# Finding the largest |w| of two weight matrices beside attention: half of the pieces on VectorE, one piece every three units, and the maximum shared through free columns of another bank

## The chip, the core and the metric

The kernel runs on one core of a Trainium2 chip. The metric is the device time of one execution in microseconds. Three runs of the kernel before gave 901.03 us (median), 900.47 and 902.3 us. The profile is of one further execution, which took 900.44 us; its span, from the first to the last recorded instruction, is 898.5 us, so 1.94 us lie outside the span.

The engines are called TensorE (PE in the rows, with PEld for its weight loads), ScalarE (ACT), VectorE (DVE), GpSimd (POOL) and SyncE (SP), which issues most transfers.

## What is computed

```python
def reference(q, k, v, n_global, n_local, x.. w_in, w_out, domain_probs, w1, w2):
    # 1. attention, 2 batches x 8 heads, 768 positions, 64 wide, a mask of a band and some global keys
    scores = q @ k.T / 8 + bias(slope of the head, distance);  a = softmax(where(keep, scores, -1e9))
    x = (a @ v) as 1536 x 512
    # 2. feed-forward, w_in 512 x 2048, w_out 2048 x 512
    h = x @ w_in;  x = (h * tanh(softplus(h))) @ w_out
    # 3. four experts, w1 512 x 1024, w2 1024 x 512 each, weighted by normalised domain_probs
    out = sum_e p[:, e] * (relu(x @ w1[e]) @ w2[e])
```

All inputs are 32-bit. The kernel computes a product of 32-bit matrices as three products of 16-bit parts: each operand is scaled by a power of two, its value rounded to 16 bits is the high part, and what is left is the low part. The scale needs the largest absolute value of the matrix, which is what the change is about.

## The kernel before, in words

**Attention.** There are 8 pairs of heads (`PAIRS`), numbered 0 to 7, and each pair has 12 units (`UNITS`): one unit is one head's block of 128 queries. A unit's number in the whole stage is 12 x pair + u, from 0 to 95. For each unit TensorE makes the scores (line 548), VectorE adds the bias and takes the row maximum (`biased`, L1122), ScalarE takes the exponential (`expo`, L858), TensorE transposes the result (`turn`, L586), ScalarE writes the high part of the transpose (L897), VectorE the low part (L1234), and TensorE multiplies with the values (`pv`, L605). ScalarE and VectorE work two units ahead with the exponentials; three buffers of scores and two banks of transposes (banks 4 and 5, one for even and one for odd units) hold the pipeline. All engines take their instructions in the written order. In units 0, 2, 4 and 6 of a pair TensorE also transposes pieces of the next pair's q and k into bank 3 (`fill`, L503), which ScalarE copies out (L848, L851). At the end of each half pair VectorE divides by the row sums (`output`, L1154, L1158, L1162). From pair 4 on, TensorE also turns a quarter of the first attention rows for the next stage (`turn_x`, L511), in units 56, 68, 80 and 87, with a high part from ScalarE (L932) and a low part from VectorE (L1219).

**The two weight matrices.** `w_in` lies in `stage`, `w_out` in `wB`, each as 8 pieces (`PIECES`) of 128 x 1024. ScalarE takes |w| of one piece with a running sum (`weights_sum`, L872; the sum bounds the maximum) in each of units 21 to 28 for `w_in` and 33 to 40 for `w_out`: a table of first units, `W_SUMS`. VectorE takes the largest of the 8 results (`weights_max`, L1082). In unit 32 or 44 (`W_SHARE`) TensorE multiplies this column with the identity into bank 3, so that each partition has all 128 values; in unit 34 or 46 (`W_SCALE`) VectorE takes their maximum (L1174) and makes the scale in a chain of four dependent operations on one column (`make_scale`, L1062 to L1065). The first fill of pairs 4 and 5 waits for that, since it writes bank 3 again.

**The splits.** GpSimd waits for the scale (`w_scale`) and then splits the 8 pieces of `w_in`, and after them the 8 of `w_out`, each in three operations: scale (L781), high part (L784), low part (L787). TensorE needs the parts of `w_in` (`w_split` at 1) from unit 93, and those of `w_out` (`w_split` at 2) before the first `second_product`.

**Feed-forward.** A step T has 12 matmuls of `first_product` (L615) and, from T = 6, 12 of `second_product` (L687) of the step T - 6. Between them an activation chain runs in order: ScalarE exponential (L975), VectorE `min` (L1351) and product (L1353), ScalarE logarithm and exponential (L991, L993), VectorE two products (L1365, L1367), GpSimd a product (L824), ScalarE high part (L985), VectorE low part (L1359). VectorE also takes the product with the bank (L1372). After T = 1 and T = 3 TensorE turns the second and third group of attention rows (16 transposes each, L511); their low parts (four times L1219) stand on VectorE after the L1372 of the same step. The second `turn_x` waits for the low parts of the first, and `second_product(0)` for those of the second.

## Time and profile before

| | value |
|---|---|
| device time, median of 3 runs | 901.03 us (900.47 to 902.3) |
| profiled execution | 900.44 us, span 898.5 us |
| TensorE matmul busy in the span | 872.5 us, 97% |
| VectorE, ScalarE, GpSimd busy | 482.7, 319.0, 260.9 us |
| chain that ended last, by engine | PE 89%, ACT 5%, DVE 3% |

The attention stage ends at about 148 us of the span and the feed-forward stage's start at about 167 us; from there TensorE is never idle for long. The slices of the page show where TensorE is less than full: the first one (start), slices 2 to 7, and the start of the feed-forward. To place a unit in the trace, take the fourth fill of a pair (`fill`, k = 3, two transposes), which stands in u = 6: unit 18 is at 39.92 us, unit 30 at 59.57, unit 42 at 80.11, unit 54 at 94.65 and unit 66 at 109.01 us.

### The profile page before, as it was taken

What the parts mean: (1) busy time and instruction counts of PE and PEld (TensorE: products, weight loads), DVE (VectorE), ACT (ScalarE), POOL (GpSimd) and SP (SyncE); (2) the same over time, 40 slices, a digit from 0 to 9 for tenths busy, and PEclk for the clock granted to TensorE, in tenths of its full rate; (3) what the DMA queues carried; (4) which work ended last, traced back from release to release, by engine and by line L of the source; (5) the groups of instructions that cost most, each with busy time, mean ns of one, the idle gap of its engine ahead of it and who ended that gap; (6) DMA issues with size and microseconds to landing.
All of it is one profiled execution on the core that took longest, in us unless ns stands there. A gap on an engine that the chain in (4) does not pass through costs nothing.

```text
span 898.5 us, 12643 instructions
## 1 busy us (share of the span) xinstructions
PE 872.5 (97%) x4918; PEld 444.0 (49%) x4918; DVE 482.7 (54%) x1008; ACT 319.0 (35%) x596; POOL 260.9 (29%) x222
## 2 busy tenths in 40 slices
PE   6988999999999999999999999999999999999998
PEld 5766876444444444444444444444444444444443
DVE  7756887999999989874442125222134321212121
ACT  4898886545554655542021010102010111101020
POOL 1659992222222222210039200077000292000000
PEclk8988999999999999999999999999999999999999
DMA  9961510000000000202100500001300000000001
GB/s 213 307 209 37 168 59 1 1 1 1 1 7 4 0 1 1 97 1 94 10 1 0 187 1 1 6 0 63 124 1 7 0 0 0 0 24 23 35 12 49
DMA packets 52004, 39.19 MB, mean 44 GB/s; under 512 B 40816, under 2 KB 41712, under 8 KB 51440
## 3 DMA queue, kind: packets, MB, share of 16 engines
q1 hardware_dynamic: 49888, 34.31, 12.9%
q10 hardware_dynamic: 2064, 4.19, 1.3%
q8 instruction: 31, 0.51, 0.2%
q14 instruction: 21, 0.17, 0.1%
HBM read 35.35 MB, written 3.15 MB: 43 GB/s over the span
## 4 chain that ended last, share of the span: by engine, by line
PE 89%; ACT 5%; DVE 3%; issue 1%; SPq 1%; DMA 0%; POOL 0%; DVEq 0%
PE bank L615 68%; PE bank L687 14%; PE bank L548 2%; PE bank L586 2%; ACT scaled L872 2%; PE bank L605 2%; ACT tmp L858 1%; ACT tmp L897 1%; PE bank L503 1%; DVE xT L1219 1%; SPq L420 1%; DMA xT<-in_v 0%; DVE tmp L1122 0%; ACT hid L848 0%; DVE tmp L1234 0%
## 5 line engine op out<-in xcount | busy, mean ns | idle before, releaser
L966 ACT ACTIVATE hid<-bank 128x512 f16<-128x512 f32 x96 | 57.3, 597 | 422.2 <-PE bank L615 422.2
L615 PE MATMUL bank<-xT,wA 128*128 128x512 f16 (+1 forms) x864 | 194.7, 379 | 0.0
L1344 DVE SCALAR_TENSOR_TENSOR hid<-bank,hid 128x512 f16<-128x512 f32 x96 | 66.4, 692 | 181.7 <-ACT hid L966 181.7
L615 PEld LDWEIGHTS bank<-xT,wA 128*128 128x128 f16 x864 | 84.4, 98 | 100.6
L687 PE MATMUL bank<-hid,wB 128*128 128x512 f16 x576 | 132.2, 379 | 0.9 <-DVE xT L1219 0.9
L615 PE MATMUL bank<-xT,wB 128*128 x576 | 125.3, 379 | 0.0
L615 PE MATMUL bank<-wB,hid 128*128 128x512 f16 x576 | 125.3, 379 | 0.0
L615 PE MATMUL bank<-wA,hid 128*128 128x512 f16 x576 | 125.3, 379 | 0.0
L824 POOL TENSOR_TENSOR tmp<-tmp 128x512 f32<-128x512 f32 x48 | 61.5, 1281 | 189.9 <-DVE tmp L1367 189.9
L781 POOL TENSOR_SCALAR stage<-stage,sc 128x1024 f32<-128x1024 f32 x32 | 36.0, 1125 | 260.4 <-DVEq L1337 250.4
L1424 DVE SCALAR_TENSOR_TENSOR acc<-bank,pg,acc 128x512 f32<-128x512 f32 x36 | 27.0, 750 | 131.7 <-PE bank L615 131.7
L687 PEld LDWEIGHTS bank<-hid,wB 128*128 128x128 f16 x576 | 56.3, 98 | 69.1 <-DVE xT L1219 1.4
L615 PEld LDWEIGHTS bank<-wA,hid 128*128 128x128 f16 x576 | 56.4, 98 | 67.9
L615 PEld LDWEIGHTS bank<-wB,hid 128*128 128x128 f16 x576 | 56.4, 98 | 68.0
L615 PEld LDWEIGHTS bank<-xT,wB 128*128 128x128 f16 x576 | 56.3, 98 | 68.0
L1234 DVE SCALAR_TENSOR_TENSOR tmp<-bank,tmp 128x384 f16<-128x384 f32 (+2 forms) x96 | 47.0, 490 | 32.8 <-ACT tmp L897 31.4
L615 PE MATMUL bank<-xT,hid 128*128 (+1 forms) x288 | 63.6, 379 | 0.0
L586 PE MATMUL bank<-ident,tmp 128*128 128x128 f32 x240 | 46.8, 296 | 8.0 <-DVE tmp L1234 5.0
L985 ACT ACTIVATE hid<-tmp 128x512 f16<-128x512 f32 x48 | 30.2, 629 | 68.0 <-POOL tmp L824 67.9
L858 ACT ACTIVATE tmp<-tmp 128x288 f32<-128x288 f32 (+2 forms) x96 | 48.5, 506 | 13.8 <-DVE tmp L1122 12.6
L615 PEld LDWEIGHTS bank<-xT,hid 128*128 128x128 f16 x288 | 28.2, 98 | 34.0
L975 ACT ACTIVATE tmp<-bank,sc 128x512 f32<-128x512 f32 x48 | 32.6, 682 | 33.4 <-PE bank L615 30.3
(113 smaller groups left out, 949.1 us busy)
## 6 DMA issues: line engine op xcount, KB each, us to landing
stage<-in_moe_w SPq DMA_DIRECT2D x8, 2048.0 KB, 9.8
stage<-in_moe_w_in SPq DMA_DIRECT2D x1, 4096.0 KB, 14.5
wB<-in_moe_w_out ACTq DMA_DIRECT2D x1, 4096.0 KB, 16.4
hid<-in_q SPq DMA_DIRECT2D x16, 192.0 KB, 3.4
hid<-in_k SPq DMA_DIRECT2D x16, 192.0 KB, 3.6
xT<-in_v SPq DMA_DIRECT2D x8, 384.0 KB, 5.1
out_y<-acc SPq DMA_DIRECT2D x12, 256.0 KB, 2.0
rows<-max SPq DMA_DIRECT2D x4, 128.0 KB, 4.3
```

Of the source, the lines that this page charges most:

```text
L586: last = pe.transpose(dst[:, b * P:(b + 1) * P], src[:, b * P:(b + 1) * P], ident[:])
L615: last = pe.matmul(dst, lhs(c, a), rhs(c, b), start=(c == 0 and n == 0), stop=(c == chunks - 1 and n == 2))
L687: last = pe.matmul(psum(4 + d), w_out_s[:, a, f // 2, f % 2, d * P:(d + 1) * P], hv[:, T % RING, b, :], start=(f == 0 and n == 0), stop=(f ...
L781: pool.tensor_scalar(tmp, src, scale, 1.0, ALU.mult, ALU.mult).then_inc(w_part, 1)
L824: pool.tensor_tensor(g_t[T % 4], g_t[T % 4], r_t[T % 2], ALU.mult).then_inc(g_ready, 1)
L858: act.activation(t, t, ACT.Exp, bias=nmax[:, u:u + 1], scale=-1.0).then_inc(p_ready, 1)
L966: act.activation(hv[:, f, 0, :], psum(f % 4), ACT.Relu).then_inc(f_hi, 1)
L975: act.activation(u_t[T % 2], psum(T % 4), ACT.Exp, scale=inv_h).then_inc(u_ready, 1)
L985: act.activation(hv[:, m % RING, 0, :], g_t[m % 4], ACT.Copy).then_inc(h_hi, 1)
L1234: dve.scalar_tensor_tensor(pt[:, 1], src, P_SCALE, pt[:, 0], ALU.mult, ALU.subtract).then_inc(pT_dve, 1)
L1344: dve.scalar_tensor_tensor(hv[:, f, 1, :], psum(f % 4), 0.0, hv[:, f, 0, :], ALU.max, ALU.subtract).then_inc(f_ready, 1)
L1424: last = dve.scalar_tensor_tensor(y, psum(4 + j), pg[:, j:j + 1], y, ALU.mult, ALU.add)
```

## The change

For each matrix the first four pieces of |w| stay on ScalarE, and the last four go to VectorE as a reduction with the largest absolute value (new function `weights_part_max`). They no longer stand in consecutive units: ScalarE takes `w_in` in units 22, 28, 34, 40 and `w_out` in 46, 52, 58, 64 (`W_ACT`), VectorE three units after each, in 25, 31, 37, 43 and 49, 55, 61, 67 (`W_DVE`). The maximum of the pieces is taken in unit 44 or 68, and shared and turned into a scale in unit 47 or 71, where TensorE writes it into columns 384 to 511 of the unit's own transpose bank, directly ahead of the transposes. The waits on bank 3 go away. (The branch for a mask that is not banded is changed too; these inputs don't take it.)

```diff
-        W_SUMS = ({0: 21, 1: 33}, {0: UNITS})
-        W_MAX = ({n: at + PIECES for n, at in W_SUMS[0].items()}, {0: UNITS + PIECES})
-        W_SHARE = ({0: 2 * UNITS + 8, 1: 3 * UNITS + 8}, {0: UNITS + 9})
-        W_SCALE = ({n: at + 2 for n, at in W_SHARE[0].items()}, {0: UNITS + 10})
+        BY_ACT, BY_DVE = range(PIECES // 2), range(PIECES // 2, PIECES)
+        W_ACT = [[2 * n * UNITS + 2 * UNITS - 2 + 6 * c for c in range(PIECES // 2)] for n in range(2)]
+        W_DVE = [[at + 3 for at in units] for units in W_ACT]
+        W_MAX = ({n: units[-1] + 1 for n, units in enumerate(W_DVE)}, {0: UNITS + 8})
+        W_SHARE = ({n: at + 3 for n, at in W_MAX[0].items()}, {0: UNITS + 9})
...
                 if banded and k == 0 and isinstance(m, int):
-                    if m in (4, 5):
-                        pe.wait_ge(w_scale, m - 3)
                     if m >= PAIRS - 2:
...
+                if banded:
+                    for n, unit in W_SHARE[0].items():
+                        if at == unit:
+                            share_max(n, psum(4 + u % 2, P, 3 * P))
                 for b in range(len((band if banded else full)[u // 2])):
                     last = pe.transpose(dst[:, b * P:(b + 1) * P], src[:, b * P:(b + 1) * P], ident[:])
...
+            def weights_part_max(n, c):
+
+                if c == BY_DVE[0]:
+                    dve.wait_ge(w_out_loaded if n else w_loaded, 16)
+                    if n:
+                        dve.wait_ge(w_max, n)
+                src = w_out_raw if n else stage
+                dve.tensor_reduce(wpieces[:, c:c + 1], src[:, c * PIECE:(c + 1) * PIECE], AX_X, ALU.max,
+                                  apply_absolute_value=True).then_inc(w_part_max, 1)
...
+            def matrix_max(n, src):
+
                 dve.wait_ge(max_psum, n + 1)
-                link(dve.tensor_reduce(scale_cols(col)[0], psum(3, P), AX_X, ALU.max))
-                make_scale(link, scale_cols(col), 10)
+                first = 2 * SCALE_STEPS + 1 + (SCALE_STEPS + 1) * n
+                chain(scale_step, first)(dve.tensor_reduce(scale_cols((SC_WIN, SC_WOUT)[n])[0], src, AX_X, ALU.max))
+
+            def matrix_scale(n):
+
+                link = chain(scale_step, 2 * SCALE_STEPS + 2 + (SCALE_STEPS + 1) * n)
+                make_scale(link, scale_cols((SC_WIN, SC_WOUT)[n]), 10)
                 dve.sem_inc(w_scale, 1)
```

ScalarE around units 21 to 24. Before, each exponential (L858) is followed by a piece (L872):

```order
65 L897 ACTIVATE tmp<-bank2 128x384 [waits pT_psum]
66 L858 ACTIVATE tmp<-tmp 128x288 [waits s_ready]
67 L872 ACTIVATE scaled,wpieces<-stage 128x1024 [waits w_sum,w_loaded]
68 L897 ACTIVATE tmp<-bank2 128x384 [waits pT_psum]
69 L858 ACTIVATE tmp<-tmp 128x128 [waits s_ready]
70 L872 ACTIVATE scaled,wpieces<-stage 128x1024 [waits w_sum]
71 L897 ACTIVATE tmp<-bank2 128x384 [waits pT_psum]
72 L858 ACTIVATE tmp<-tmp 128x128 [waits s_ready]
73 L872 ACTIVATE scaled,wpieces<-stage 128x1024 [waits w_sum]
```

After, in the same place of the program (L905 is what was L897, L864 what was L858, L880 the piece):

```order
65 L905 ACTIVATE tmp<-bank2 128x384 [waits pT_psum]
66 L864 ACTIVATE tmp<-tmp 128x288 [waits s_ready]
67 L905 ACTIVATE tmp<-bank2 128x384 [waits pT_psum]
68 L864 ACTIVATE tmp<-tmp 128x128 [waits s_ready]
69 L880 ACTIVATE scaled,wpieces<-stage 128x1024 [waits w_sum,w_loaded]
70 L905 ACTIVATE tmp<-bank2 128x384 [waits pT_psum]
71 L864 ACTIVATE tmp<-tmp 128x128 [waits s_ready]
72 L905 ACTIVATE tmp<-bank2 128x128 [waits pT_psum]
73 L864 ACTIVATE tmp<-tmp 128x256 [waits s_ready]
```

One piece stands where three stood; the next follows six units later.

VectorE at the end of pair 3. Before, the scale of `w_out` is made in unit 46 (row 208 is that unit's low part):

```order
208 L1234 SCALAR_TENSOR_TENSOR tmp<-bank2,tmp 128x384 [waits pT_act]
209 L1174 TENSOR_REDUCE sc<-bank1 128x1 [waits max_psum]
210 L1062 TENSOR_SCALAR sc<-sc 128x1 [waits scale_step]
211 L1063 TENSOR_SCALAR sc<-sc 128x1 [waits scale_step]
212 L1064 TENSOR_SCALAR sc<-sc 128x1 [waits scale_step]
213 L1065 TENSOR_SCALAR sc<-sc 128x1 [waits scale_step]
214 L1162 TENSOR_TENSOR acc<-bank3,tmp 128x384 [waits scale_step,o_step]
```

After, what stands there is the scale of `w_in`, in unit 47, around that unit's low part (L1265):

```order
207 L1179 TENSOR_TENSOR acc<-bank3,tmp 128x384 [waits o_step]
208 L1139 ISA tmp<-bank0,tmp 128x128 [waits s_psum]
209 L1139 ISA tmp 128x1
210 L1191 TENSOR_REDUCE sc<-bank2 128x1 [waits max_psum,pT_act]
211 L1265 SCALAR_TENSOR_TENSOR tmp<-bank2,tmp 128x384 [waits scale_step]
212 L1068 TENSOR_SCALAR sc<-sc 128x1
213 L1069 TENSOR_SCALAR sc<-sc 128x1 [waits scale_step]
214 L1070 TENSOR_SCALAR sc<-sc 128x1 [waits scale_step]
215 L1071 TENSOR_SCALAR sc<-sc 128x1 [waits scale_step]
```

The scale of `w_in` has moved from unit 34 to unit 47, and that of `w_out` from unit 46 to unit 71. GpSimd's own list of instructions is the same in both kernels; its first split waits for the scale of `w_in`.

## Rows read from the trace of the kernel before

**Rows 1.** Windows, one per pair: start:end, us, busy (x count) by engine, granted clock, DMA.

```profile
39.92:59.57 19.65, 16.35 (x176) 13.27 (x173) 11.01 (x42) 19.11 (x45) 15.82 (x23) 0.83 0.85 264
59.57:80.11 20.54, 16.68 (x175) 13.59 (x175) 11.96 (x49) 19.33 (x45) 12.51 (x9) 0.83 0.17 39
80.11:94.65 14.54, 13.61 (x174) 11.30 (x174) 12.11 (x49) 11.85 (x29) 14.03 (x11) 1.00 0.25 57
94.65:109.01 14.36, 13.78 (x179) 11.48 (x176) 11.71 (x43) 12.27 (x30) 13.66 (x11) 1.00 0.60 175
```

**Rows 2.** Timeline, attention: start, us, engine, line, operation, tiles [idle before <-releaser].

```profile
44.24 1.04 ACT L872 ACTIVATE scaled<-stage 128x1024 f32<-128x1024 f32 x1
...
45.18 0.19 ACT L872 ACTIVATION_READ_ACCUMULATOR scaled<-stage 128x1 f32 x1
...
92.60 0.53 ACT L858 ACTIVATE tmp<-tmp 128x288 f32<-128x288 f32 x1
...
93.94 0.52 PE L586 MATMUL bank<-ident,tmp 128*128 128x128 f32 x3
...
101.82 0.40 ACT L858 ACTIVATE tmp<-tmp 128x128 f32<-128x128 f32 x1 [1.22 <-DVE tmp L1122]
```

**Rows 3.** Timeline of VectorE: the chain, unit 47's low part, and a reduction.

```profile
85.49 0.28 DVE L1174 TENSOR_REDUCE sc<-bank 128x1 f32<-128x128 f32 x1
...
87.34 0.55 DVE L1234 SCALAR_TENSOR_TENSOR tmp<-bank,tmp 128x384 f16<-128x384 f32 x1
...
180.13 1.21 DVE L1072 TENSOR_REDUCE wpieces<-stage 128x1 f32<-128x1024 f32 x1
```

**Rows 4.** Timeline of GpSimd: first split of each matrix, first feed-forward product.

```profile
67.09 1.12 POOL L781 TENSOR_SCALAR stage<-stage,sc 128x1024 f32<-128x1024 f32 x1 [9.97 <-DVEq L1176]
...
102.71 1.13 POOL L781 TENSOR_SCALAR scaled<-wB,sc 128x1024 f32<-128x1024 f32 x1
...
153.51 1.27 POOL L824 TENSOR_TENSOR tmp<-tmp 128x512 f32<-128x512 f32 x1 [14.31 <-DVE tmp L1367]
```

**Rows 5.** Timeline at the start of the feed-forward, VectorE and TensorE.

```profile
149.16 0.43 DVE L1351 TENSOR_SCALAR tmp<-tmp 128x512 f32<-128x512 f32 x1 [0.82 <-ACT tmp L975]
...
149.95 5.34 PE L615 MATMUL bank<-xT,wA 128*128 128x512 f16 x24
...
152.74 0.69 DVE L1367 SCALAR_TENSOR_TENSOR tmp<-xT,tmp 128x512 f32<-128x512 f32 x1
...
153.95 2.47 DVE L1219 TENSOR_TENSOR xT<-bank,xT 128x512 f16<-128x512 f32 x4
...
156.57 1.94 PE L511 MATMUL bank<-ident,acc 128*128 128x128 f32 x16 [1.28 <-DVE xT L1219]
...
158.34 7.93 PE L615 MATMUL bank<-xT,wA 128*128 128x512 f16 x36
...
167.20 2.76 PE L687 MATMUL bank<-hid,wB 128*128 128x512 f16 x12 [0.93 <-DVE xT L1219]
```

**Rows 6.** Timeline, later stretches: VectorE and GpSimd at the same time.

```profile
174.95 1.27 POOL L824 TENSOR_TENSOR tmp<-tmp 128x512 f32<-128x512 f32 x1 [3.47 <-DVE tmp L1367]
...
175.39 1.11 DVE L1351 TENSOR_SCALAR tmp<-tmp 128x512 f32<-128x512 f32 x1
...
301.88 1.27 POOL L824 TENSOR_TENSOR tmp<-tmp 128x512 f32<-128x512 f32 x1 [3.46 <-DVE tmp L1367]
...
302.31 1.38 DVE L1294 SCALAR_TENSOR_TENSOR xT<-acc,sc,xT 128x512 f16<-128x512 f32 x1
...
605.69 1.12 POOL L781 TENSOR_SCALAR stage<-stage,sc 128x1024 f32<-128x1024 f32 x1
...
605.91 0.93 DVE L1401 TENSOR_SCALAR pg<-pr,sc 128x4 f32<-128x4 f32 x1
```

**Rows 7.** Windows of 4 us, same columns: TensorE's clock after a wait.

```profile
50.00:54.00 4.00, 2.58 (x14) 2.02 (x13) 1.60 (x8) 4.00 (x10) 3.67 (x6) 0.62 1.08 385
54.00:58.00 4.00, 4.00 (x31) 3.36 (x27) 2.19 (x7) 4.00 (x10) 2.89 (x5) 0.53 0.53 130
```

More of the change, by code:

```diff
@@ L550, in scores_of_two, with share_max @@
                             last.then_inc(s_psum, 1)
-            def share_max(n):
+            def share_max(n, dst=psum(3, P)):
                 pe.wait_ge(w_max, n + 1)
-                pe.matmul(psum(3, P), wpart[:, 0:1].to_broadcast([P, P]), ident[:], start=True, stop=True
+                pe.matmul(dst, wpart[:, 0:1].to_broadcast([P, P]), ident[:], start=True, stop=True
                           ).then_inc(max_psum, 1)
@@ L907, in pair @@
                         load_w_out()
-                    for n, start in W_SUMS[0 if banded else 1].items():
-                        if at - start in range(PIECES):
-                            if n and at == start:
-                                act.wait_ge(w_max, n)
-                            weights_sum(n, at - start)
+                    for n in range(2 if banded else 1):
+                        units = W_ACT[n] if banded else W_FULL
+                        if at in units:
+                            weights_sum(n, units.index(at))
                     if at + 1 in V_SUMS:
@@ L921, in pair @@
                     load_w_out()
-                    act.wait_ge(w_max, 1)
-                    for c in range(PIECES):
+                    for c in BY_ACT:
                         weights_sum(1, c)
@@ L1168, in first @@
                     biased(0, 0, 1, banded)
[L1170 to L1172 removed]
+            def matrix_max(n, src):
                 dve.wait_ge(max_psum, n + 1)
[L1174 to L1175 removed]
+                first = 2 * SCALE_STEPS + 1 + (SCALE_STEPS + 1) * n
[3 more added lines that the diff above has]
+                make_scale(link, scale_cols((SC_WIN, SC_WOUT)[n]), 10)
                 dve.sem_inc(w_scale, 1)
             def matrix_step(m, u, banded):
[L1181 to L1186 removed]
+                at = m * UNITS + u
+                for n in range(2 if banded else 1):
+                    units = W_DVE[n] if banded else W_FULL
+                    if at in units:
+                        weights_part_max(n, BY_DVE[units.index(at)])
+                    if at == W_MAX[0 if banded else 1][n]:
+                        weights_max(n)
+                    if banded and at == W_SHARE[0][n]:
+                        matrix_scale(n)
+                if not banded and at == W_SCALE_FULL:
+                    matrix_max(0, psum(3, P))
+                    matrix_scale(0)
             def values_low():
@@ L1232, in pair @@
                     dve.wait_ge(pT_act, base + u + 1)
+                    if banded:
+                        for n, unit in W_SHARE[0].items():
+                            if (2 * i + slot) * UNITS + u == unit:
+                                matrix_max(n, psum(4 + u % 2, P, 3 * P))
                     src, pt = p_out(u, banded)
@@ L1444, in _ @@
                 dve.sem_inc(tables_free, 1)
+                for c in BY_DVE:
+                    weights_part_max(1, c)
                 weights_max(1)
-                matrix_scale(1, SC_WOUT)
+                matrix_max(1, psum(3, P))
+                matrix_scale(1)
                 rest()
```

19 lines of the change are left out of this document (9 added, 10 removed).

## The prediction

> **What bounds the kernel now.** I read the slices first: TensorE is full from 167 us to the end, so a gain must come from the stages ahead of that, and what counts is when TensorE starts `second_product(0)`, at 167.20 us [rows 5]. Everything behind it follows one for one. Next I cut attention into windows, one per pair, from fourth fill to fourth fill [rows 1]. The two windows that hold the 16 pieces take 19.65 and 20.54 us, and ScalarE is busy for 19.11 and 19.33 us of them: it is the bound there, each piece being 1.04 + 0.19 us of its time [rows 2]. The windows without pieces take 14.54 and 14.36 us with TensorE busy for 13.6 and 13.8: TensorE is the bound, with ScalarE at 11.9 to 12.3 and VectorE at 11.7 to 12.1 us. Third, the timeline from 148 to 167 us [rows 5]: VectorE goes from L1351 at 149.16 to L1367 at 152.74, then L1372 and four L1219 that end at 156.42, and only then may TensorE turn x again, having waited since 155.29 (149.95 + 5.34). VectorE is the bound of this stretch. Fourth, GpSimd's timeline [rows 4]: it starts to split at 67.09, takes 35.62 us for `w_in` (to 102.71), and is done at 139.20 (153.51 less an idle time of 14.31), 72.1 us after its start and 10 us ahead of that VectorE chain.
>
> **What attention gains.** A pair without pieces, scale or x costs about 13.6 us: the window from 94.65 (14.36) less 0.44 us of `turn_x` on TensorE and a third of a microsecond for L1219; TensorE's busy time of 13.61 in the third window is the floor. From unit 18 (39.92) to unit 54 (94.65) there are 54.73 us; three such pairs are 40.8, so 13.9 us are extra. Two scale chains are in it, at 14.54 - 13.6 = 0.9 us each; the 16 pieces cost 12.1 us, 0.75 us each.
>
> After the change a piece stands alone. On ScalarE it takes 1.23 us, on VectorE 1.21 us, by the same kind of reduction [rows 3]. What of it reaches TensorE depends on the lead: an exponential ends at 93.13 and its transpose starts at 93.94 [rows 2], a lead of 0.8 us, so 0.4 to 0.5 us of a lone piece come through. Four of ScalarE's pieces (u = 10) fall close to the pair's end, where it waits 1.22 us for VectorE anyway [rows 2]; against that, VectorE's pieces in u = 1 come when it is late already. Bounds: 0.2 us each if only busy time counts (11.85 + 2 x 1.23 = 14.3 against 13.6 is 0.7 us for a pair's four pieces), 0.75 us as today. I take 0.45, nearest to the lead's row. The scale chains now stand after unit 47's and unit 71's low part, at the pair's end where VectorE is late, and one of them behind an L1219: 1.1 us each. Extra time after: 16 x 0.45 + 2 x 1.1 = 9.4 us. **Attention ends 13.9 - 9.4 = 4.5 us earlier.** The shared matmul (0.24 us of TensorE's time) stays; the waits of two fills on bank 3 go, and the fills stood at pair ends which VectorE holds back all the same, so I give nothing for them.
>
> **What it costs: GpSimd starts late.** The split waits for the scale of `w_in`, now in unit 47. Before, unit 42's fill is at 80.11 and unit 47's low part at 87.34 [rows 3], 7.2 us later with a chain of 0.9 ahead of it, so 6.3 without. After: 39.92 + 2 x 13.6 + 9 pieces x 0.45 + 6.3 = 77.5; the maximum (0.28), the low part (0.55) and the chain with its signal (1.1; before, all this but the low part went from 85.49 to about 86.6) give 79.4. GpSimd starts 12.3 us later than at 67.09 and is done, if undisturbed, at 139.2 + 12.3 = 151.5. The scale of `w_out` (unit 71, some 112 us) is in time for 79.4 + 35.6 = 115.0. TensorE's use of the `w_in` parts from unit 93 on (136 us or later) is covered too, and `w_out`'s parts are needed only at 167. The transfers of the first expert's weights, which SyncE issues behind `w_split`, move to 115 us and have 50 us of room.
>
> But VectorE's chain L1351 to L1367 now begins at 149.16 - 4.5 = 144.7, while GpSimd is still splitting, 6.8 us long. In the trace the two collide [rows 6]: L1351 beside a GpSimd product takes 1.11 us and not 0.43; L1294, with two inputs in SBUF, takes 1.38 and ends 0.54 us after GpSimd's operation ends; a TENSOR_SCALAR of only four elements takes 0.93 us and ends 0.03 us after GpSimd's L781. So VectorE operations of these two kinds wait until the GpSimd operation is over. The Trainium skill (SBUF — State Buffer, "SBUF: two separate sides") calls this an exclusive lock on a shared port pair, taken by whoever starts first and held for the whole instruction; all three pairs of rows agree with it.
>
> L1351, L1353, L1351, L1353, L1365, L1367 are all of these kinds; L1372 and L1219 read one input from PSUM and are not. I lay them out against GpSimd's operations of 1.12, 1.05 and 2.13 us, taking turns. GpSimd's last four operations start, undisturbed, at 144.8 (2.13), 147.1, 148.3 and 149.4 (2.13). VectorE: L1351 waits to 144.8, ends 145.2; GpSimd to 147.3; L1353 to 148.0; GpSimd to 149.1, with L1372 under it; L1351 to 149.5; GpSimd to 150.6; L1353 to 151.3; GpSimd to 153.4, its last; L1365 to 154.0, L1367 to 154.7. Before, L1367 ended at 153.4. **The 4.5 us are gone, and VectorE is 1.3 us later than before.** In general, a piece cheaper by 0.1 brings attention forward by 1.6 us but GpSimd's end by only 0.9 us, and it is GpSimd's end that now sets this point: L1367's end is 150.65 + 9 x (cost of a piece), 152.5 for 0.2 and 157.4 for 0.75.
>
> **And TensorE cools down.** The four L1219 now end at 156.4 + 1.3 = 157.7, but TensorE has done its 24 matmuls at 155.3 - 4.5 = 150.8: it idles for 6.9 us where it idled for 1.28. Attention shows what follows a thin stretch: in 50 to 54 us, with TensorE 65% busy after the waits for ScalarE, the granted clock is 0.62, and in 54 to 58 us, with TensorE busy throughout, 0.53 [rows 7], near the lower of its two levels (1.2 against 2.4 GHz). Read as a share of time at half clock, the two rows make 3.0 + 3.8 = 6.8 us, some 5.5 of them work. I take 5.5 us of work at half speed, 2.75 us lost; the bounds are nothing and all 6.8 us, 3.4 lost. TensorE then needs 1.77 us for the 16 transposes (156.57 to 158.34), 7.93 for 36 matmuls and the 2.75, and is at `second_product(0)` at 157.7 + 0.15 + 12.45 = 170.3. Before it was 167.2, of which 0.93 was a wait for VectorE, so the loss of the clock is hidden for that much. The result is **+3.1 us**: 903.5 for a profiled execution like the one at 900.44, 904.1 on the median of 901.03.
>
> **The rivals.**
> (a) The collision costs little: the splits' operations leave VectorE its turn, or VectorE's reads pass beside them. Against it stand all of [rows 6]. Then only GpSimd's first product is late: ready at 149.0, started at 151.5, 2.5 us, of which 1.3 are slack (ScalarE's exponential of T = 1 ended at 156.7, VectorE used it at 158.0). Gain 4.5 - 1.2 = 3.3 us: 897.7. Chance 0.14. The skill's lock is what speaks against this one.
> (b) Collision as forecast, but TensorE keeps its clock or regains it at once: VectorE's 1.3 us is all, 902.3. For it: 97% busy around. Against: a wait of 6.9 us is longer than any inside attention. Chance 0.18.
> (c) The pieces are nearly hidden (0.2 us each or less): GpSimd starts 2.3 us earlier, result 3.1 - 9 x 0.25 = +0.8, 901.9. For it: the pieces' positions. Chance 0.13.
> (d) The pieces cost as much as today, 0.7, because VectorE has no lead to spare either: attention gains 0.5, and the result is 3.1 + 9 x 0.25 = +5.4, 906.4. Chance 0.12.
> The forecast itself, between (c) and (d) with the clock lost, has 0.43.
>
> **How the numbers follow.** Predicted 904.1 us. The range must reach from near (a) to (d): 899 to 907 leaves out most of (a) and a little above (d). A measurement of this kernel can tell about 0.2%, 1.8 us, from no change: faster is below 899.2, slower above 902.8. Slower: forecast 0.42, (d) 0.12, part of (b) 0.06, together 0.60. Same: (b) 0.12, (c) 0.12, 0.01 of each of two others, together 0.26. Faster: (a), 0.14.
>
> **What the profile would show.** Windows of the pairs 1 to 5 at 15 to 16 us with the clock at 1.00 throughout (pieces at 0.45); one at 14 speaks for (c), one above 16.5 for (d). GpSimd's first split at 79 to 80 us, its last one ending after 152. L1351, L1353, L1365 and L1367 of the first two steps longer than 0.43 and 0.69 us, each ending shortly after a GpSimd operation; if they keep their times, (a). TensorE's idle time ahead of its second group of L511 near 7 us, and a clock of about 0.5 behind it; if 1.00, (b). The forecast is wrong if L1367's first end is earlier than 153 us, or if the feed-forward later loses or regains time behind 170 us, where I expect none.

## The result, and the profile after

The changed kernel takes 902.46 us (median of 22 executions, 901.21 to 903.93); the kernel before, run beside it, takes 900.69. The ratio is 1.0013, 95% interval 1.0007 to 1.0019: 1.2 us slower by the ratio and 1.8 by the medians, small but clear of the noise, within the 0.2% that the prediction calls no change, and inside the forecast range. The profiled execution took 903.18 us, 2.7 more than the profiled one of before (900.44); the first is the third slowest of its 22 and the second the third fastest of its 22, so this pair shows more than the typical difference.

In these two executions the whole difference lies ahead of `second_product(0)`: TensorE starts it at 169.79 against 167.20, 2.59 us later, and from there to the end of the span both need 731.3 to 731.4 us.

Windows of the changed kernel, one per pair (units 18 to 78, from fourth fill to fourth fill), columns as in [rows 1]:

```profile
40.26:55.30 15.04, 13.61 (x176) 11.10 (x173) 11.97 (x42) 13.35 (x33) 13.80 (x20) 1.00 0.98 324
55.30:70.83 15.53, 13.65 (x172) 11.12 (x173) 13.15 (x45) 13.55 (x33) 2.02 (x4) 1.00 0.30 69
70.83:87.71 16.88, 13.91 (x175) 11.39 (x175) 14.13 (x51) 13.48 (x33) 7.79 (x6) 1.00 0.21 48
87.71:103.67 15.96, 14.27 (x176) 11.67 (x177) 13.66 (x46) 14.04 (x34) 15.36 (x12) 1.00 0.23 52
103.67:121.46 17.79, 15.81 (x178) 13.00 (x178) 13.91 (x52) 12.17 (x30) 17.01 (x13) 0.90 0.27 99
```

The two windows of 19.65 and 20.54 us are gone, and ScalarE is no longer full in any. The five windows come to 81.20 us; before, from 39.92 to unit 78's fill at 123.37, they came to 83.45, so these units take 2.25 us less. Unit 18, ahead of which no piece lies, came 0.34 us later in this execution (40.26), which leaves attention 1.9 us ahead at unit 78, not 4.5. The last window has a granted clock of 0.90. The windows of 4 us show where:

```profile
112.00:116.00 4.00, 2.65 (x27) 2.35 (x28) 2.98 (x17) 2.46 (x6) 3.92 (x3) 0.92 0.00 0
116.00:120.00 4.00, 4.00 (x31) 3.24 (x31) 2.23 (x8) 2.35 (x7) 3.73 (x4) 0.66 0.81 286
```

Then the end of attention, timeline of GpSimd and VectorE together (L1350 is before's L1319; L1382, L1384, L1396, L1398, L1403 are L1351, L1353, L1365, L1367, L1372; L787 to L793 are L781 to L787, the three operations of a split; L1246 is L1219), to be held against [rows 4, 5]:

```profile
79.58 1.12 POOL L787 TENSOR_SCALAR stage<-stage,sc 128x1024 f32<-128x1024 f32 x1 [22.11 <-DVEq L1197]
...
144.97 2.13 POOL L793 TENSOR_TENSOR wB<-scaled,wB 128x1024 f16<-128x1024 f32 x1
147.20 1.12 POOL L787 TENSOR_SCALAR scaled<-wB,sc 128x1024 f32<-128x1024 f32 x1
148.41 1.09 POOL L790 TENSOR_SCALAR wB<-scaled 128x1024 f16<-128x1024 f32 x1
149.59 2.45 POOL L793 TENSOR_TENSOR wB<-scaled,wB 128x1024 f16<-128x1024 f32 x1
```

```profile
146.10 1.02 DVE L1350 TENSOR_TENSOR sc<-sc 128x1 f32<-128x1 f32 x1
147.15 0.16 DVE L1351 TENSOR_TENSOR sc<-sc 128x1 f32<-128x1 f32 x1
148.13 0.48 DVE L1382 TENSOR_SCALAR tmp<-tmp 128x512 f32<-128x512 f32 x1 [0.81 <-ACT tmp L981]
148.64 1.40 DVE L1384 SCALAR_TENSOR_TENSOR tmp<-tmp 128x512 f32<-128x512 f32 x1
150.08 0.69 DVE L1403 SCALAR_TENSOR_TENSOR tmp<-bank,tmp 128x512 f32<-128x512 f32 x1
150.68 1.63 DVE L1382 TENSOR_SCALAR tmp<-tmp 128x512 f32<-128x512 f32 x1
152.35 0.69 DVE L1384 SCALAR_TENSOR_TENSOR tmp<-tmp 128x512 f32<-128x512 f32 x1
152.96 0.69 DVE L1396 SCALAR_TENSOR_TENSOR xT<-tmp 128x512 f32<-128x512 f32 x1
153.68 0.69 DVE L1398 SCALAR_TENSOR_TENSOR tmp<-xT,tmp 128x512 f32<-128x512 f32 x1
```

GpSimd starts 12.5 us later than before and is still at work when attention ends. L1350, one column that takes 0.15 us alone, takes 1.02 and ends at 147.12, 0.02 after GpSimd's product (147.10). It stands ahead of ScalarE's exponential, so of the 1.9 us by which attention is ahead only 1.0 is left when the chain starts (148.13 against 149.16). L1384 takes 1.40 in place of 0.69 and ends 0.54 after GpSimd's L790; L1382 takes 1.63 in place of 0.43 and ends 0.27 after GpSimd's last operation (152.04). Operations behind 152.04 have their old times. L1403, which reads a bank of PSUM, has its 0.69 beside GpSimd. So the chain's last end is 154.37 against 153.43 before.

The timeline of TensorE behind it, and its clock:

```profile
148.04 5.34 PE L621 MATMUL bank<-xT,wA 128*128 128x512 f16 x24
157.51 3.64 PE L513 MATMUL bank<-ident,acc 128*128 128x128 f32 x16 [4.12 <-DVE xT L1246]
160.94 9.02 PE L621 MATMUL bank<-xT,wA 128*128 128x512 f16 x36
```

```profile
152.00:156.00 4.00, 1.38 (x7) 0.41 (x5) 3.93 (x7) 2.24 (x5) 1.30 (x2) 1.00 0.00 0
156.00:160.00 4.00, 2.49 (x12) 2.52 (x13) 3.93 (x8) 2.19 (x4) 0.00 (x0) 0.54 0.02 6
160.00:164.00 4.00, 4.00 (x16) 2.08 (x15) 3.60 (x6) 2.24 (x4) 1.27 (x1) 0.61 0.00 0
```

TensorE waits for 4.12 us where it waited for 1.28, and the granted clock falls to 0.54 and 0.61, near the lower of its two levels. The 16 transposes take 1.70 us longer than before and the 36 matmuls 1.09; the wait of 0.93 that stood ahead of `second_product(0)` is gone. 0.94 + 2.79 - 0.93, less 0.2 by which the groups of matmuls overlap in the rows, is the 2.59.

### The profile page after: what moved, and what is told of

Its sections match the earlier page's. It is cut to its first block, busy times and chain, and to the rows that moved or that the text cites. A ratio compares the mean times of both kernels' runs of the same rounds, so it can differ in the third digit from the quotient of the medians.

```text
span 901.2 us, 12640 instructions
## 1 busy us (share of the span) xinstructions
PE 872.5 (97%) x4918; PEld 443.6 (49%) x4918; DVE 493.3 (55%) x1016; ACT 311.2 (35%) x580; POOL 261.3 (29%) x222
## 4 chain that ended last, share of the span: by engine, by line
PE 88%; DVE 5%; ACT 5%; issue 2%; POOL 0%; DVEq 0%
PE bank L621 68%; PE bank L693 14%; ACT tmp L864 2%; PE bank L550 1%; ACT tmp L905 1%; PE bank L592 1%; PE bank L611 1%; DVE tmp L1139 1%; ACT scaled L880 1%; DVE wpieces L1088 1%; PE bank L505 1%; PE bank L569 1%; DVE tmp L1265 1%; DVE xT L1246 1%; PE bank L513 1%
## 5 line engine op out<-in xcount | busy, mean ns | idle before, releaser
L787 POOL TENSOR_SCALAR stage<-stage,sc 128x1024 f32<-128x1024 f32 x32 | 36.0, 1125 | 272.6 <-DVEq L1368 250.4
L1265 DVE SCALAR_TENSOR_TENSOR tmp<-bank,tmp 128x384 f16<-128x384 f32 (+2 forms) x96 | 47.0, 490 | 21.3 <-ACT tmp L905 19.3
L864 ACT ACTIVATE tmp<-tmp 128x288 f32<-128x288 f32 (+2 forms) x96 | 48.4, 505 | 18.9 <-DVE tmp L1139 18.1
```

The costliest lines, as they stand in the source:

```text
L787: pool.tensor_scalar(tmp, src, scale, 1.0, ALU.mult, ALU.mult).then_inc(w_part, 1)
L864: act.activation(t, t, ACT.Exp, bias=nmax[:, u:u + 1], scale=-1.0).then_inc(p_ready, 1)
L1265: dve.scalar_tensor_tensor(pt[:, 1], src, P_SCALE, pt[:, 0], ALU.mult, ALU.subtract).then_inc(pT_dve, 1)
```

## The experiments

The kernels of experiments 1 to 4, 5 to 8, 9 and 10, and 11 and 12 were each run beside the kernel before on one chip; its medians there were 901.14, 900.62, 900.75 and 900.99, and the ratios below are against it. "Changed" is the changed kernel.

**1. The collision alone: before, with GpSimd made late.**

```diff
             pool.wait_ge(w_scale, 1)
+            pool.wait_ge(pT_dve, 44)
```

> The kernel before, with one more wait: GpSimd, when it has the scale of w_in, also waits until VectorE has written the low part of unit 43 (pT_dve at 44, some 81.5 us). Attention's own work is as before. Theory (collision): the split ends, undisturbed, near 81.6 + 72.1 = 153.7 us, 4.5 us into VectorE's chain that begins at 149.16; L1351 and L1353 of the first steps grow beyond 0.43 and 0.69 us, L1367's first end moves from 153.4 to 156 or later, TensorE waits 4 to 5 us ahead of its second group of transposes and its clock falls; second_product(0) moves from 167.2 to 171 to 172 us, the kernel takes 4 to 5 us more (905). Rival (no collision, only a late start of GpSimd's first product): the split ends where the first product starts anyway, 153.5 us, so the time stays within 1 us of 900.7.

904.82 us, ratio 1.0039 (1.0027 to 1.0051). GpSimd's first split came at 83.55 and its last operation ended at 155.90. Timelines of VectorE and TensorE:

```profile
149.40 1.61 DVE L1320 TENSOR_TENSOR sc<-sc 128x1 f32<-128x1 f32 x1
...
152.51 1.40 DVE L1354 SCALAR_TENSOR_TENSOR tmp<-tmp 128x512 f32<-128x512 f32 x1
```

```profile
161.38 3.19 PE L511 MATMUL bank<-ident,acc 128*128 128x128 f32 x16 [4.70 <-DVE xT L1220]
```

With nothing of the change but a late start (3.9 us later than in the changed kernel, at GpSimd's end), the same operations are long by the same amounts, L1354 by 1.40 and the second L1352 by 1.63, TensorE waits 4.70 us, and its clock falls (0.73 in 160 to 164 us; the transposes take 3.19 us and not 1.94). The ratio makes it 3.5 us. `second_product(0)` came 5.4 us later than before in the profiled execution, 1.4 of which were there at unit 42 already (fill at 81.49 against 80.11), before GpSimd's first split. The collision is a cause of its own.

**2. The collision away: the changed kernel with GpSimd's last two pieces of `w_out` set to zero and not split** (that part of the output's work is left out).

```diff
+                if c < PIECES - 2: split(...)
+                else: pool.memset(hi, 0.0); pool.memset(lo, 0.0)
```

> The kernel after, but GpSimd fills the parts of w_out's last two pieces with zeros (memset) in place of splitting them, so its work ends some 7 to 9 us earlier, near 143 to 145 us, before VectorE's chain begins at 148 us; the feed-forward is computed with a part of w_out missing. Nothing else changes. Theory (collision): L1382 and L1384 (before: L1351, L1353) are back at 0.43 and 0.69 us, L1398's first end moves from 154.4 to 151.5 us, TensorE's wait ahead of its second group of transposes falls from 4.1 to about 1.3 us, the clock stays at 1.00, and second_product(0) starts at 165.3 in place of 169.8: 898.7 us, 2 us faster than before. Rival (the late feed-forward start has another cause, such as TensorE's clock alone): it stays at 169 to 170 and the time at 902 to 903.

898.39 us, ratio 0.9962 (0.9946 to 0.9977). GpSimd is done at 145.98 and VectorE's chain has its old durations:

```profile
146.93 0.43 DVE L1386 TENSOR_SCALAR tmp<-tmp 128x512 f32<-128x512 f32 x1 [0.81 <-ACT tmp L985]
```

```profile
154.33 1.94 PE L513 MATMUL bank<-ident,acc 128*128 128x128 f32 x16 [1.27 <-DVE xT L1250]
```

Without GpSimd beside the chain the change would be a gain of 2.7 us by the medians. The loss hangs on GpSimd's row, and attention's gain is real.

**3. The clock away: 16 spare matmuls for TensorE between its `first_product` and its wait.**

```diff
+                    if T == 3:
+                        pe.wait_ge(b_ready, 1)
+                        for _ in range(16):
+                            pe.matmul(psum(0), w_in_s[:, 0, 0, 0:P], xs(0, 0, 0), start=True, stop=True)
```

> The kernel after with 16 spare matmuls of 512 columns on TensorE behind the first_product of T = 3, in the time in which it waits for VectorE (4.1 us; the 16 take 3.5 us at full clock), into a bank that is free. Results are not touched. Theory (part of the loss is TensorE's clock after that wait): the granted clock stays at 1.00 in 156 to 164 us, the second group of transposes takes 1.8 us and not 3.4, and second_product(0) starts at 168.1, bounded by VectorE, 1.7 us earlier than 169.8; the time falls by 1.7 us against after, to 900.8 to 901.4. Rival (the clock is hidden, VectorE's chain is the bound all the way): second_product(0) stays at 169.8.

901.09 us, ratio 0.9998 (0.9988 to 1.0007). Windows of two pairs, timeline of TensorE, and that of VectorE:

```profile
54.97:70.50 15.53, 13.64 (x173) 11.12 (x173) 13.16 (x45) 13.54 (x33) 2.00 (x4) 1.00 0.31 69
...
103.32:119.54 16.22, 14.26 (x179) 11.82 (x179) 13.84 (x52) 12.27 (x30) 15.53 (x12) 1.00 0.22 68
```

```profile
151.29 3.62 PE L747 MATMUL bank<-xT,wA 128*128 128x512 f16 x16
156.64 1.94 PE L513 MATMUL bank<-ident,acc 128*128 128x128 f32 x16 [1.74 <-DVE xT L1250]
...
167.27 2.77 PE L693 MATMUL bank<-hid,wB 128*128 128x512 f16 x12 [0.92 <-DVE xT L1250]
```

```profile
145.46 1.49 DVE L1386 TENSOR_SCALAR tmp<-tmp 128x512 f32<-128x512 f32 x1 [0.81 <-ACT tmp L985]
146.98 1.49 DVE L1388 SCALAR_TENSOR_TENSOR tmp<-tmp 128x512 f32<-128x512 f32 x1
...
149.11 0.54 DVE L1386 TENSOR_SCALAR tmp<-tmp 128x512 f32<-128x512 f32 x1
149.68 2.50 DVE L1388 SCALAR_TENSOR_TENSOR tmp<-tmp 128x512 f32<-128x512 f32 x1
...
152.81 0.69 DVE L1402 SCALAR_TENSOR_TENSOR tmp<-xT,tmp 128x512 f32<-128x512 f32 x1
```

The clock stayed at 1.00, here and, by itself, at 112 to 120 us as well, where the code is the changed kernel's. So this execution shows both sums clean: attention's five windows take 79.60 us, a gain of 3.85, VectorE's chain starts 3.7 us earlier than before, and it ends at 153.50 against 153.43. In it the first L1386 loses 1.06 us, the first L1388 0.80, the second L1386 0.12 and the second L1388 1.81: 3.8 in all. All that attention gained is eaten by the collision, to 0.1 us.

**4. GpSimd early: the table with pieces every two units at times, `w_in` done at unit 35.**

```diff
+        W_ACT = [[21,25,29,33],[40,46,52,58]]
+        W_DVE = [[23,27,31,35],[43,49,55,61]]
+        W_MAX = ({0: 36, 1: 62}, {0: UNITS + 8})
+        W_SHARE = ({0: 39, 1: 64}, {0: UNITS + 9})
```

> The kernel after with another table: w_in's pieces every two units from 21 (ScalarE 21, 25, 29, 33, VectorE 23, 27, 31, 35), its maximum in 36 and its scale in 39, in the middle of a pair; w_out's pieces every three units from 40 (ScalarE 40, 46, 52, 58, VectorE 43, 49, 55, 61), maximum in 62, scale in 64, also mid-pair. Theory: the pieces cost about 0.5 us each as in after (7.7 to 8.5 us in all), the two chains, which in after cost 1.4 us (unit 47) and 3.0 us (unit 71) at pair ends, cost 0.3 each in the middle where VectorE has time; attention ends 4.5 to 5.5 us earlier than before. GpSimd starts at 65 to 67 us and ends by 139, so nothing collides at 143 us: second_product(0) at 162 to 163 us, the kernel at 896 us (895.5 to 897.5). Rival (chains cost the same anywhere, or pieces every two units cost 0.75 as in before): attention ends 1 to 2.5 us earlier, 898 to 900 us.

900.15 us, ratio 0.9986 (0.9977 to 0.9995): a little better than before, but I had expected far more. GpSimd started at 71.92, ended at 144.83, and nothing collided. But the first two windows took 17.03 and 19.00 us:

```profile
39.63:56.66 17.03, 13.82 (x175) 11.22 (x172) 13.08 (x43) 13.36 (x33) 15.65 (x23) 1.00 0.98 314
56.66:75.66 19.00, 14.24 (x178) 11.54 (x174) 14.10 (x51) 14.56 (x35) 3.71 (x5) 0.99 0.19 42
```

Less the bare pair of 13.6 that is 0.7 us for each of five pieces, and, if the scale chain costs 1.4 here too, 1.0 for each of four; what the chain costs in mid-pair was not measured by itself. A piece two units behind another costs as much as one in a row of ScalarE's did, or more. The third window had its clock down (0.82) and took 17.69. VectorE's last chain began at 150.14, 1 us later than before and not 4 earlier, and that is where the gain from the missing collision went.

**5. The shared maximum of `w_in` back in bank 3.**

```diff
+                    if m == 5:
+                        pe.wait_ge(w_scale, 1)
-                        if at == unit:
+                        if n and at == unit:
```

> The kernel after with one part undone: the maximum of w_in (not of w_out) is shared through bank 3 again, by a matmul behind unit 45, and the first fill of the next pair (unit 48) waits for the scale; VectorE still takes its maximum and makes the scale in unit 47. Theory (the chain's cost is VectorE's time at the pair's end, the bank matters little): the pair from unit 42 to 54 takes 16.9 us as in after, plus at most 0.4 us for the fill that waits; the time is that of after within 0.5 us. Rival (the waits on bank 3 were a part of what the change gains): the pair takes 1 us more or longer, the kernel 903.5 or more.

901.80 us, ratio 1.0017 (1.0006 to 1.0028), the changed kernel's within 0.7. The window from unit 42's fill was 1.2 us longer in the profiled execution, as the rival had it, but with a granted clock of 0.72 at 78 to 84 us. So what the free columns are worth by themselves is not settled; by the times it is small.

**6. What VectorE's pieces cost: the changed kernel without its eight reductions** (their maxima are set to 0).

```diff
-                dve.tensor_reduce(wpieces[:, c:c + 1], src[...], AX_X, ALU.max, ...)
+                dve.memset(wpieces[:, c:c + 1], 0.0)
```

> The kernel after with VectorE's eight pieces left out (zeros in their place, so the scales rest on half of each matrix); ScalarE's eight stay where they are. One look at attention. Theory (a lone piece costs about 0.47 us on either engine): the pairs from unit 18, 30, 42 and 54 take 0.5 to 1 us less each than in after (15.4, 15.5, 16.9, 16.0): near 14.7, 14.6, 15.9, 15.0. Rival (ScalarE's pieces are hidden by its waits at pair ends, VectorE's cost it all): 13.8, 13.7, 15.1, 14.5. Rival (VectorE's are hidden): as in after.

One execution, 900.20 us, which the time alone can't be judged by. Windows of two pairs:

```profile
54.61:69.18 14.57, 13.44 (x173) 11.02 (x173) 11.20 (x45) 13.44 (x33) 2.41 (x4) 1.00 0.34 78
69.18:85.16 15.98, 13.68 (x175) 11.29 (x175) 12.16 (x51) 13.44 (x33) 7.38 (x6) 1.00 0.23 52
```

Two reductions fewer make the first 0.96 us shorter than in experiment 3: 0.48 us each. Between these two windows lies a scale chain, 15.98 - 14.57 = 1.4 us. VectorE's last chain now begins at 142.52, 6.6 us earlier than before, and ends at 151.43 beside GpSimd (done at 150.16): only 2.0 us of 6.6 are left. GpSimd's end sets this point, as the prediction's sum has it.

**7. The scale of `w_in` three units earlier.**

```diff
+        W_ACT = [[21,27,33,39],[45,51,56,61]]
+        W_DVE = [[24,30,36,42],[48,53,58,63]]
+        W_MAX = ({0: 42, 1: 63}, {0: UNITS + 8})
+        W_SHARE = ({0: 44, 1: 65}, {0: UNITS + 9})
```

> The kernel after with another table: pieces still one every three units, but from unit 21 on (w_in: ScalarE 21, 27, 33, 39, VectorE 24, 30, 36, 42), its scale in unit 44 and not 47; w_out's from 45 (ScalarE 45, 51, 56, 61, VectorE 48, 53, 58, 63), its scale in unit 65, in the middle of a pair, and not in 71. Theory (GpSimd's end sets the start of the feed-forward, and chains at a pair's end cost 1.4 us and a fall of the clock): GpSimd starts near 75.5, not 79.3, and ends near 148 us; pieces cost 0.47 each as in after, the chains 0.3 to 0.9, so VectorE's chain begins near 144 us (5 us earlier than before), collides for 4 us, and L1398's first end is near 150.5 to 151 us, 2.5 us earlier than before; the clock does not fall at 112 us. If the clock also holds in the wait of some 3.5 us ahead of the second transposes, 898.2 us; if it falls there, 899.9. Rival (attention's end alone counts): 895.7 us. Rival (GpSimd's end does not matter, as VectorE waits for something else): no better than after, 902.

903.55 us, ratio 1.0030 (1.0018 to 1.0041), a clear miss. GpSimd ended at 150.65, ahead of the chain, but attention lost more than that gave:

```profile
55.82:72.95 17.13, 14.03 (x173) 11.27 (x173) 12.89 (x44) 13.32 (x33) 0.80 (x3) 1.00 0.21 47
```

This window holds four pieces, three units apart, as does the one of 15.53. From 55.5 to 72.9 us ScalarE waits 3.5 us for VectorE's L1139, in six units, against 1.7 us in three in the changed kernel. Where a piece stands within the pair matters as much as how many there are. `second_product(0)` began at 169.81, as late as in the changed kernel, here without a collision.

**8. The same with 12 spare matmuls** (the edit of experiment 3, 12 for 16).

> e6_scale_44 with 12 spare matmuls of 512 columns (2.6 us) on TensorE behind the first_product of T = 3. Theory (clock): the granted clock is 1.00 from there on in every execution, so the slower ones of e6 go: 898.2 us and a narrower spread. Rival (the clock holds by itself, or the spare work delays the transposes): equal to e6 or slower by up to 1 us.

904.06 us, ratio 1.0031 (1.0019 to 1.0044). Nothing to win: in experiment 7's profiled execution the clock at the start of the feed-forward was 1.00 already. Of the two kernels that got spare matmuls, they paid in the one whose clock had fallen there.

**9. Parity or place: the changed table moved two units earlier.**

```diff
+        W_ACT = [[20,26,32,38],[44,50,56,62]]
+        W_DVE = [[23,29,35,41],[47,53,59,65]]
+        W_MAX = ({0: 42, 1: 66}, {0: UNITS + 8})
+        W_SHARE = ({0: 45, 1: 69}, {0: UNITS + 9})
```

> The changed kernel with its whole table of pieces moved two units earlier: ScalarE's at units 20, 26, 32, 38 and 44, 50, 56, 62, VectorE's at 23, 29, 35, 41 and 47, 53, 59, 65, the two chains at 45 and 69. Spacing and the split between the engines stay as they are; ScalarE's pieces stay at even units and VectorE's at odd ones, but they stand at other places of the head pair (ScalarE 8 and 2, VectorE 11 and 5 in place of 10 and 4, 1 and 7). It asks why the run with pieces at 21, 27, 33, 39 had a second window of 17.13 us against 15.53. Theory A, that it is the parity (which engine's piece falls on the even units): this table costs what the changed kernel's costs, the window from unit 30's fill to unit 42's stays near 15.5, GpSimd starts its splits two units (2.6 us) earlier, near 77.0, and ends near 149.4, so that about half of the collision with VectorE's chain goes; 901.4, 1.0 under the changed kernel in the same call. Theory B, that it is the place in the pair: windows near 17, GpSimd from 78.5 on, and 903.5.

902.93 us, ratio 1.0022 (1.0014 to 1.0031). The second window is 16.34 us, GpSimd starts at 79.05, only 0.5 earlier than in the changed kernel though its signal stands two units earlier. The parity is as in the changed kernel and the window is 0.8 us longer, so the place counts, as theory B has it; but 16.34 lies halfway between 15.53 and 17.13, so the place alone is shown for half of that difference. Here TensorE itself waits longer (2.2 us for L1139 and 2.1 for L1265 between 40 and 72 us, against 0.6 each in the changed kernel); which unit's neighbours make a place cheap I have not found out.

**10. Two of GpSimd's pieces held back.** Pieces 6 and 7 of `w_out` are read only from `second_product(12)` on.

```diff
+            HELD = {4: PIECES - 2, 8: PIECES - 1}
+            for c in range(PIECES - len(HELD)):
+                w_out_piece(c)
             pool.sem_inc(w_split, 1)
             for T in range(STEPS):
                 pool.wait_ge(q_ready, T + 1)
                 pool.tensor_tensor(g_t[T % 4], g_t[T % 4], r_t[T % 2], ALU.mult).then_inc(g_ready, 1)
+                if T in HELD:
+                    w_out_piece(HELD[T])
...
+                    if g == 0 and f in (FT - 4, FT - 2):
+                        pe.wait_ge(w_out_part, f // 2 + 1)
```

> The changed kernel with GpSimd's last two pieces of w_out not split before the first feed-forward products but behind GpSimd's products of steps 4 and 8, while the matmuls of the second product that read them wait for them at steps 12 and 14. Nothing is left out. GpSimd's row of splits should end near 143.0 (152.0 less two pieces of 4.5), ahead of VectorE's chain at the end of attention (145.5 to 148.1). My theory says that the collision there is what ate the attention's gain: the chain runs in 4.3 us, TensorE's second turn waits about 1.3 us instead of 4.1, and the time is that of the run whose last two pieces were only zeroed, 898.4, plus what the two pieces cost where they now lie. There VectorE is busy 94% of the time and TensorE all of it; a piece lengthens VectorE's operations beside it by some 2.3 us and GpSimd's next product comes up to 1.3 us late, but first product and second product run six steps apart and that slack should take both: 898.6. Rival: the slack doesn't hold, since VectorE has only 0.3 us in 5 to catch up with, and each piece costs TensorE 2.3 us: 903.0.

901.61 us, ratio 1.0011 (1.0001 to 1.0020). The first half came as expected: the chain ran undisturbed and TensorE was at `second_product(0)` at 166.16, 3.6 us earlier than in the changed kernel. Then VectorE beside a held piece, and TensorE later on:

```profile
174.34 1.11 DVE L1389 TENSOR_SCALAR tmp<-tmp 128x512 f32<-128x512 f32 x1
175.49 1.49 DVE L1391 SCALAR_TENSOR_TENSOR tmp<-tmp 128x512 f32<-128x512 f32 x1
176.90 1.52 DVE L1397 TENSOR_TENSOR hid<-tmp,hid 128x512 f16<-128x512 f32 x1
178.34 2.61 DVE L1403 SCALAR_TENSOR_TENSOR xT<-tmp 128x512 f32<-128x512 f32 x1
```

```profile
PE bank L695 <- ACT acc L963: 2.3, 1, 2.3
...
PE bank L621 <- DVE tmp L1410: 0.7, 1, 0.7
```

(the second fence lists TensorE's waits from 145 to 260 us: engine, tile and line, whom it waited for, us in total, times, longest). Three operations cost 0.80, 0.83 and 1.92 us more than alone: 3.6 us a piece, not my 2.3. VectorE has almost no idle time there: counted from `second_product(0)`, its L1391 comes 3.1 us later than L1353 did before behind the first piece and 6.3 behind the second, and stays so to 268 us. Of this TensorE pays 0.67 us at 205.86 and 2.3 near 252, where ScalarE copies `x2` out only after its steps' exponentials. The cost was moved, and 3.0 of the 3.6 us were lost again.

**11. One piece held back** (`HELD = {4: PIECES - 1}`, and the one wait at `f == FT - 2`).

> The changed kernel with only GpSimd's last piece of w_out held back behind its product of step 4; the matmuls that read it wait at step 14. With two held pieces VectorE's chain ran undisturbed and second_product(0) began at 166.16 against 169.79, but each held piece cost VectorE 3.6 us where it then lay, and TensorE later lost 0.67 us (205.86) and 2.3 us (near 252). Theory A: VectorE lags by 3.6 us in place of 7.1, which the three steps between a product and the reuse of its bank cover, so both later waits vanish; GpSimd's row ends at 147.5, VectorE's chain starts between 145.5 and 148.1 and loses at most 1 us; 902.0 (the changed kernel's median in this call, near 902.5) less 3.0 is 899.4. Rival B: the collision that is left takes it all, since the chain starts beside GpSimd's last two operations: second_product(0) at 168 or later, 901.5.

899.72 us, ratio 0.9984 (0.9975 to 0.9993). Theory A holds: GpSimd's row ends at 146.60, the chain starts at 145.40 and loses 1.1 us, `second_product(0)` begins at 165.00, and neither later wait is there.

**12. One piece held back, and the second chain at unit 69.**

```diff
+        W_DVE = [[25, 31, 37, 43], [49, 55, 61, 65]]
+        W_MAX = ({0: 44, 1: 66}, {0: UNITS + 8})
+        W_SHARE = ({0: 47, 1: 69}, {0: UNITS + 9})
```

> As the kernel with one held piece, and the second scale chain two units earlier: VectorE's last piece of w_out at unit 65 in place of 67, its maximum at 66 in place of 68, the shared maximum and the chain at 69 in place of 71. It asks for the cause of the fall of the granted clock at 112 to 120 us, which the profiled runs of the changed kernel and of two variants have and the run with spare matmuls (the same code up to there) and the run with the table two units earlier (chain at 69) don't have. Theory A, that the fall comes from this chain standing at unit 71 behind an x_low: it is gone here, the window from unit 66's fill to unit 78's is 16.2 us or less against 17.8, and the time is 898.0. Rival B, that it comes and goes between executions wherever the chain stands: time as with one held piece alone, within 0.8.

898.59 us (898.17 to 899.16 in 7 executions), ratio 0.9972 (0.9960 to 0.9983). It beats both kernels: 2.4 us less than before. Its window of units 66 to 78, and TensorE's wait behind the chain in the changed kernel (unit 71) and here (unit 69):

```profile
103.71:119.68 15.97, 14.31 (x179) 11.88 (x179) 13.86 (x52) 12.24 (x30) 15.38 (x11) 1.00 0.22 63
```

```profile
113.63 0.84 PE L550 MATMUL bank<-hid 64*128 64x256 f32 x8 [1.06 <-DVE tmp L1139]
```

```profile
110.86 0.70 PE L550 MATMUL bank<-hid 64*128 64x256 f32 x4 [0.73 <-DVE tmp L1146]
```

At unit 71 the L1246, the shared maximum and the chain follow each other within one unit; at unit 69 the chain is through before L1253 comes. The longest wait is 0.3 us shorter and the clock is kept. In the profiled executions with the chain at unit 71 the clock fell there in some (changed, experiments 2 and 10) and not in others (3, 5, 6, 11), and in neither with the chain at 69 (9, 12). With other tables it fell elsewhere in attention: to 0.83 at 104 to 108 us in experiment 7, to 0.82 over units 42 to 54 in experiment 4. The median is 1.1 us under experiment 11's, between the 1.7 of theory A and none of B, and its executions lie within 1.0 us where those of experiment 11 lie within 2.3. The two profiled executions don't show the 1.1 us: both begin `second_product(0)` at 165.0. All this speaks for the place of the chain as a cause and doesn't prove it.

## Why the prediction was right, and where it was off

**The outcome against the forecast.** The forecast was 904.1 and gave slower (above 902.8) a chance of 0.60 and same 0.26; 902.46 is in the range, and on the side that it held less likely. Its path (GpSimd late, a collision that takes attention's gain, a wait that costs the clock) is what the runs show; several sizes on it are not.

**What GpSimd does: right.** First split at 79.4 forecast, 79.58 measured; end if undisturbed 151.5, measured 152.04 with 0.3 of it from the collision. The point on which the case turns, that GpSimd's row now reaches into the chain at the end of attention, held, and experiments 1, 2 and 6 show it as a cause, not as a coincidence. Rival (a) is out: had VectorE its turn, L1384 would have kept 0.69. The Trainium skill (SBUF — State Buffer, "SBUF: two separate sides") describes such a lock for the whole of an instruction; these rows agree, down to L1350's 1.02 us for a single column, and, as shown below, on GpSimd's side too.

**The pieces: right.** 0.45 forecast; 0.48 for VectorE's by difference (experiment 6) and 0.48 for all four of a window against a bare pair ((15.53 - 13.6) / 4). The bare pair is the forecast's own figure, and no run left ScalarE's pieces out. That the value hangs on the place within the pair the forecast did not see: 0.9 at experiment 7's places ((17.13 - 13.6) / 4).

**The scale chains: undersized.** 1.1 forecast, 1.3 to 1.4 measured (16.87 - 15.53 in experiment 3's windows, 15.98 - 14.57 in experiment 6). Twice 0.2 to 0.3 us is most of the difference between 4.5 and the 3.85 us that attention gains with its clock kept.

**The clock inside attention: missed.** The forecast had 1.00 throughout. In the profiled execution it fell to 0.66 behind the chain at unit 71, 17.79 against 16.22 us in experiment 3, 1.6 us. The gain over the five windows was then 2.25, and 1.9 by the time of unit 78. I had priced the chain but not looked at what a wait of 1.06 us in a pair that already waits would do.

**The collision: the term of the sum that was mis-sized.** I forecast a chain that starts 4.5 us earlier and ends 1.3 later, so a collision that costs 5.8 us; experiment 3 measured 3.8. I let the two engines take turns with GpSimd waiting for each VectorE operation in full, twice 0.4 and twice 0.7 us less the gaps, so its last operation would end 1.9 us late at 153.4 and L1367 at 154.7. In experiment 3 the turns are as forecast, but GpSimd's three operations take 1.17, 1.35 and 2.18 against 1.12, 1.04 and 2.13 alone: 0.4 us in all (their starts, at 146.76, 148.01 and 149.45, say the same against 142.20, 143.40 and 144.53). It ends at 151.63 and the chain at 153.50. What I missed is that a turn overlaps at both ends. GpSimd in experiment 3:

```profile
146.76 1.17 POOL L791 TENSOR_SCALAR scaled<-wB,sc 128x1024 f32<-128x1024 f32 x1
...
148.01 1.35 POOL L794 TENSOR_SCALAR wB<-scaled 128x1024 f16<-128x1024 f32 x1
...
149.45 2.18 POOL L797 TENSOR_TENSOR wB<-scaled,wB 128x1024 f16<-128x1024 f32 x1
```

L794 starts while L1388 still has 0.46 us to run (to 148.47) and takes 0.31 more; L791 and L797 start with 0.2 to go and take 0.05 more; in the changed kernel L793 starts with 0.45 to go and takes 0.32 more. So GpSimd also waits until VectorE's operation is over, less some 0.14 us (an estimate from these differences); in the same way a VectorE operation of 0.69 ends only 0.54 after GpSimd's. A turn of VectorE's therefore costs GpSimd 0.05 to 0.3 us, while a wait for one of GpSimd's long operations costs VectorE up to 2. I also left out that L1319, ahead of the chain, collides: 0.13 us in experiment 3, 0.87 in the changed kernel.

**TensorE's wait: too long, the cost of the clock right.** 6.9 us forecast, 4.12 measured, since attention ended 2.6 us later than forecast while GpSimd's end came out near it. The cost of the clock, 2.75 us, came out as 2.79, and 0.93 of it was hidden as forecast. Rival (b), that the clock is kept, is what experiment 3 shows when it is helped: 901.09.

**The total.** For an execution like the profiled one the forecast was +3.1 and the measured difference +2.7. That is partly luck, since two errors cancelled in it: attention was 1.9 us ahead and not 4.5, and the collision cost 2.8 us (1.9 + 0.94) and not 5.8. VectorE's end (1.3 forecast, 0.94 measured) would have been near 0.1 had attention kept its clock. Over all executions the change costs 1.2 us by the ratio (1.8 by the medians), less than forecast, and before's median was 900.69 and not the 901.03 that the forecast started from. Since the executions of both kernels lie 2.4 to 2.7 us apart, and falls of the clock come and go in attention between profiled ones, the median very likely takes in executions that lose less than this one did. How many keep their clock at which place the times alone do not tell. Behind 170 us no time was lost or regained, as forecast.

## What to carry to other kernels

Work that is moved to free one engine also moves the start of whoever waits for its result: follow that engine to its new end, and see what it stands beside there. Here it was cheaper to put off one piece of GpSimd's work, which is not read until `second_product(14)`, than to make everything earlier. A filler instruction has no price of its own: 0.48 us at one place of a pair, 0.9 one unit over, and a scale chain costs 1.4 at one place and, in some executions behind another step of VectorE's, a fall of the clock as well.

## What the runs showed of the hardware

- A VectorE TENSOR_TENSOR of one column, 0.15 us alone, took up to 1.61 us beside GpSimd (experiment 1). Size doesn't protect an operation. Operations that read a bank of PSUM were not longer (L1403, 0.69 in both), nor were VectorE's reductions of a piece (1.21 us beside GpSimd's splits at 97.06 us of the changed kernel, 1.21 at 64.22 with GpSimd idle).
- Both engines wait for each other, and the cost is uneven because GpSimd's operations are the longer ones: VectorE's 0.69 became 1.40 to 2.61, GpSimd's 1.04 at most 1.35 and its 2.13 at most 2.45. GpSimd's loss was each time what VectorE's operation still had to run, less about 0.14 us (0.45 and 0.31, 0.30 and 0.17, 0.20 and 0.05; experiments 1, 3, 10).
- TensorE's granted clock fell to 0.92 and 0.66 at 112 to 120 us behind waits of 0.20, 0.37 and 1.06 us, in some executions of the same code and not in others (1.00 in experiments 3 and 11, with the same waits).
- Nor did the length of one wait decide it. Ahead of the second turn of x the transposes were slow behind waits of 2.50, 4.12 and 6.65 us (3.53 to 3.65 us; experiment 11, changed, 6) and at full speed behind 2.79 and 3.37 (1.94 us; experiments 12 and 9).
